# Windowed attention feeding a routed MoE: x turned between the two pairs of turned probabilities, and another tail of the routing

## The reference

```python
scores = scale * np.matmul(q, k.transpose(0, 1, 3, 2))
keep = is_sink | in_window                    # pos < 4, or 0 <= rel < 128
a = softmax(np.where(keep, scores, -1e9))
x = np.matmul(a, v)                           # then [3072 tokens, 512]

logits = x @ w_gate                           # [3072, 8]
expert_idx = np.argmax(logits, axis=1)
gate_w = softmax(logits)[expert_idx]
out[mask] = gate_w[mask, None] * (np.maximum(x[mask] @ w1[e], 0.0) @ w2[e])   # for each expert e

h = out @ w_in
result = (h - np.tanh(h)) @ w_out
```

## Time and profile before

| | us |
|---|---|
| median of three runs | 1124.79 (1124.62 to 1126.35) |
| the profiled execution, whole | 1124.74 |
| its span, first to last instruction | 1123.0 |
| passes of attention, start of the span to the last pass's scores | about 180 |
| tail of the routing, to the first product of stage two | 180 to 203.6 |
| stages two and three | 203.6 to 1123 |
| TensorE busy in the whole span | 1089.1 |

### The profile page before, as it was taken

One profiled execution on the slowest core, in us unless ns is written; L12 is line 12 of the kernel. 1 busy time (PEld: TensorE's weight loads), 2 busy tenths in 40 slices (PEclk: granted clock), 3 DMA queues, 4 the chain that ended last, 5 costly groups with the idle time before them and its releaser, 6 DMA issues.

```text
span 1123.0 us, 17069 instructions
## 1 busy us (share of the span) xinstructions
PE 1089.1 (97%) x5993; PEld 875.9 (78%) x5993; DVE 610.1 (54%) x1326; ACT 478.3 (43%) x1016; POOL 492.7 (44%) x494
## 2 busy tenths in 40 slices
PE   9999998899999999999989999999999999999995
PEld 6777775688888888888867888888888888888884
DVE  6787686222232223223258666666666666666664
ACT  7788874414133414442444333333333333333331
POOL 3256525707025436482274345335335335435432
PEclk9999998999999999999999999999999999999998
DMA  8636723524215344464231100001010010001000
GB/s 274 194 125 211 247 82 123 179 94 161 74 52 192 93 151 141 150 203 144 90 109 58 37 10 38 19 20 39 10 29 38 1 38 38 1 1 38 1 1 38
DMA packets 37916, 99.44 MB, mean 89 GB/s; under 512 B 8272, under 2 KB 8400, under 8 KB 32720
## 3 DMA queue, kind: packets, MB, share of 16 engines
q1 hardware_dynamic: 29392, 52.30, 14.9%
q0 software_dynamic: 8448, 46.17, 11.8%
HBM read 75.84 MB, written 22.61 MB: 88 GB/s over the span
## 4 chain that ended last, share of the span: by engine, by line
PE 91%; DVE 3%; POOL 2%; issue 2%; DMA 1%; ACT 1%; SPq 0%; POOLq 0%; DVEq 0%; ACTq 0%
PE bank L668 22%; PE bank L660 22%; PE bank L596 14%; PE bank L610 14%; PE bank L426 5%; PE bank L460 4%; PE bank L442 3%; PE bank L602 2%; PE bank L583 1%; PE bank L492 1%; DVE x_tok L951 1%; PE bank L648 1%; PE bank L504 1%; POOL sq L1376 1%; DMA qT<-qt 0%
## 5 line engine op out<-in xcount | busy, mean ns | idle before, releaser
L1286 POOL TENSOR_TENSOR weights<-raw,weights 128x1024 fp32r<-128x1024 f32 x72 | 171.3, 2401 | 201.2 <-ACT weights L716 200.0
L660 PE MATMUL bank<-mT_hi,weights 128*128 128x512 f32 x768 | 253.0, 391 | 1.9 <-DVE mT_lo L1113 1.9
L668 PE MATMUL bank<-weights,gT_hi 128*128 128x512 f32 x768 | 241.8, 396 | 6.9 <-DVE gT_lo L1170 6.7
L1375 POOL TENSOR_SCALAR ser<-ser 128x512 f32<-128x512 f32 x96 | 64.0, 666 | 288.1 <-DVE ser L1152 288.0
L668 PEld LDWEIGHTS bank<-weights,gT_hi 128*128 128x128 f32 x768 | 142.2, 189 | 41.1 <-DVE gT_lo L1170 12.7
L660 PEld LDWEIGHTS bank<-mT_hi,weights 128*128 128x128 f32 x768 | 145.0, 189 | 32.4 <-DVE mT_lo L1113 2.1
L668 PE MATMUL bank<-weights,gT_lo 128*128 128x512 f32 x384 | 150.5, 392 | 0.0
L660 PE MATMUL bank<-mT_lo,weights 128*128 128x512 f32 x384 | 150.1, 391 | 0.0
L596 PE MATMUL bank<-weights,mT_hi 128*128 128x512 f32 x464 | 147.8, 400 | 1.5 <-issue 1.5
L610 PE MATMUL bank<-weights,hT_hi 128*128 128x512 f32 x464 | 148.7, 401 | 0.0
L859 ACT ACTIVATE bank<-bank 128x512 f32<-128x512 f32 x96 | 55.9, 582 | 214.0 <-DVE ser L1162 214.0
(11 more groups left out here) (141 smaller groups left out, 1575.6 us busy)
## 6 DMA issues: line engine op xcount, KB each, us to landing
raw<-w_all POOLq DMA_DIRECT2D x32, 1024.0 KB, 5.6
raw<-w_all SPq DMA_DIRECT2D x8, 1024.0 KB, 6.5
sorted_y<-ys SPq DMA_DIRECT2D x30, 257.0 KB, 3.3
xs<-sorted_x SPq DMA_DIRECT2D x29, 257.0 KB, 2.8
kT<-kt SPq DMA_DIRECT2D x24, 264.0 KB, 2.9
qT<-qt SPq DMA_DIRECT2D x24, 256.0 KB, 3.3
v_in<-vt SPq DMA_DIRECT2D x24, 256.0 KB, 3.7
raw<-sorted_y SPq DMA_DIRECT2D x20, 257.0 KB, 2.7
```

Of the source, the lines that this page charges most:

```text
L660: done = e.matmul(bank[HB[n % 3]][:, :], wt[:, f // 2, c, cols], x[:, c, :], start=(c == 0 and m == 0), stop=(c == CH - 1 and m == 2))
L668: done = e.matmul(bank[YB[i]][:, :], x[:, n % 3, rows], wt[:, f, :], start=(f == 0 and m == 0), stop=(f == GCH - 1 and m == 2))
L1286: e.tensor_tensor(lo, src, hi.bitcast(F32), ALU.subtract).then_inc(s_w_lo, 1)
L1375: e.tensor_scalar(row, row, SERIES_2, 1.0, ALU.mult, ALU.add).then_inc(s_ser, 1)
```

## The change

- On TensorE `turn_prob(i, 0)` now stands ahead of `turn_x(w)`, and `turns` follows: `turn_prob(i, 1)` waits for the reader of `turn_prob(i, 0)`, and `turn_x` has its bank from pair 3 of the tile before. VectorE copies `part(i, 0)` ahead of `normalise(w)`.
- The start of each expert's region is added by one more small product in `rank` (`region_b`), not by a step on VectorE; `places` has three steps where it had four.
- The logits are negated when ScalarE copies them, so the maximum becomes a minimum. For the last three sets, of one tile each, `pick` has four steps where it had five, `tally` is left out (`rank` adds the one-hot rows of those tiles by products), and the exponential's sum is taken by ScalarE.
- The ranks of the last three sets have PSUM banks of their own (1, 2, 3), and the logits of the last tile go to bank 6. The wait of `small_bank_read` for them falls away, and `rank` stands where its input is due.
- VectorE's list behind the last pass is written out: the copy of pair 2 first, then `pick`, `gates`, `places` of the single tiles around `add_logits`.
- ScalarE normalises x of the last two tiles, eight activations of 128x64 each with the row's factor as a pointer.
- Of the products that nobody reads, the two are gone, the five stand ahead of the last rank, and 32 stand where 18 stood. Behind the turn of the first slot 11 transposes of the identity are new.

```diff
@@ turns @@
+        if i < ALL:
+            turns += [("prob", i, 0)]
         if 0 <= w < ALL:
             turns += [("x", w, 0)]
         if i < ALL:
-            turns += [("prob", i, 0), ("prob", i, 1)]
+            turns += [("prob", i, 1)]
@@ banks @@
+        def logits_bank(w):
+            return bank[O_BANK] if w == ALL - 1 else bank[R_BANK]
+        def rank_of(b):
+            tiles = SETS[b][1]
+            bk = bank[R_BANK] if b < MULTI else bank[1 + b - MULTI]
+            return bk[:, 0:tiles * E].rearrange("p (t e) -> p t e", t=tiles)
+        def norm_on_act(w):
+            return w >= ALL - 2
@@ tensor: rank @@
+                    for g in range(SETS[MULTI][0], start):
+                        e.matmul(rk, ones[:, :], hot_all[:, g:g + 1, :], start=False, stop=False, skip_group_check=True)
+                e.matmul(rk, ones[:, :], region_b[:, :].unsqueeze(1).broadcast_to([P, tiles, E]),
+                         start=False, stop=True, skip_group_check=True).then_inc(s_rank, 1)
@@ tensor: the passes @@
-                if 0 <= w < ALL:
+                if 0 <= w < ALL - 1:
                     small_bank_read(w)
+                if i == ALL:
+                    rank(MULTI)
                 if 0 <= w < ALL:
                     logits(w)
+                if i < ALL:
+                    turn_prob(i, 0)
+                if 0 <= w < ALL:
                     turn_x(w)
-                if w == ALL - 1:
-                    keep_warm(2)
                 if sinks:
                     sink_values(g)
-                if i < ALL:
-                    turn_prob(i, 0)
+                if i == ALL + 1:
+                    rank(MULTI + 1)
                 if 0 <= w < ALL:
                     turn_logits(w)
-                if i == ALL + 2:
-                    keep_warm(5)
-                if i - 3 in LAST:
-                    rank(LAST.index(i - 3))
+                    if i - 3 in LAST:
+                        rank(LAST.index(i - 3))
+            keep_warm(5, bank[0])
+            rank(MULTI + 2)
...
-            keep_warm(18)
+            keep_warm(32, bank[R_BANK])
@@ tensor: behind the turn of the first slot @@
             turn_slot_x()
+            for _ in range(11):
+                e.transpose(bank[R_BANK][:, 0:P], ident[:, :], ident[:, :])
@@ scalar @@
+            def normalise(w):
+                e.wait_ge(s_rinv, w + 1)
+                e.wait_ge(s_x_turned, w + 1)
+                b = set_of[w - RING_X]
+                e.wait_ge(scattered[b], 16 * SETS[b][1])
+                bk = bank[T_OF[turn_at["x", w, 0] % 2]]
+                for h in range(H):
+                    cols = slice(h * D, (h + 1) * D)
+                    done = e.activation(x_tok[:, w % RING_X, cols], bk[:, cols], ACT.Copy, scale=rinv[:, w % 2, h:h + 1])
+                done.then_inc(s_norm_act, 1)
@@ vector: a pass @@
+                part(i, 0)
-                if 0 <= w < ALL:
+                if w >= 0:
                     normalise(w)
-                if i < ALL:
-                    part(i, 0)
```

More of the change, by code:

```diff
@@ L470, in small_bank_read @@
                 b = next((n for n in range(NSETS) if LAST[n] == w - 2), None)
-                if b is not None:
-                    e.wait_ge(s_place, 3 * b + 1)
+                if b is not None and b < MULTI:
+                    e.wait_ge(s_place, 2 * b + 1)
             def turn_sinks(g):
@@ L1035, in routing_of, with at_once @@
             def routing_of(i):
-                new = LAST.index(i - 3) if i - 3 in LAST else None
-                old = LAST.index(i - 4) if i - 4 in LAST else None
-                if new is not None:
-                    yield from pick(new)
-                if old == NSETS - 1:
-                    e.wait_ge(s_counts, 1)
-                    e.tensor_tensor(tail_rows[:, :], bank[0][:, 0:E], region[:, 0, :], ALU.add).then_inc(s_tail_rows, 1)
-                if old is not None:
-                    yield from places(old)
-                if new is not None:
-                    if new < NSETS - 1:
-                        yield from tally(new)
-                    yield from gates(new)
+                if i - 3 in LAST:
+                    yield from pick(LAST.index(i - 3))
+                if i - 4 in LAST:
+                    yield from places(LAST.index(i - 4))
+                if i - 3 in LAST:
+                    yield from tally(LAST.index(i - 3))
+                    yield from gates(LAST.index(i - 3))
+            def at_once(steps):
+                for _ in steps:
+                    pass
             e.memset(mask[:, :, :, :], 0.0).then_inc(c_zero, 1)
@@ L1054, in vector @@
             e.wait_ge(c_mask0, 1)
-            for i in range(ALL + 4):
+            for i in range(ALL):
                 g, w = i - 1, i - 2
-                in_values = 0 <= g < ALL
                 routing = routing_of(i)
@@ L1062, in vector @@
                     e.wait_ge(c_parted, 2)
-                    e.wait_ge(c_region, 2)
-                if i >= ALL:
-                    for _ in routing:
-                        pass
+                    e.wait_ge(c_region, 3)
                 for h in range(H):
-                    if i < ALL:
-                        masked_max(i, h)
-                    if h == 0 and 0 <= w < ALL:
+                    masked_max(i, h)
+                    if h == 0 and w >= 0:
                         invert(w)
-                    if h == 3 and in_values:
+                    if h == 3 and g >= 0:
                         for p in (2, 3):
@@ L1076, in vector @@
                     next(routing, None)
-                if 0 <= w < ALL:
+                part(i, 0)
+                if w >= 0:
                     normalise(w)
-                if i < ALL:
-                    part(i, 0)
-                if 0 <= w < ALL:
                     add_logits(w)
-                if i < ALL and not part_on_act(i, 1):
+                if not part_on_act(i, 1):
                     part(i, 1)
-                for _ in routing:
-                    pass
-                if i < ALL and i % TILES == 1:
+                at_once(routing)
+                if i % TILES == 1:
                     sink_values_lo(i // TILES)
+            part(ALL - 1, 2)
+            at_once(pick(MULTI))
+            at_once(places(MULTI - 1))
+            at_once(gates(MULTI))
+            at_once(places(MULTI))
+            invert(ALL - 2)
+            add_logits(ALL - 2)
+            at_once(pick(MULTI + 1))
+            at_once(gates(MULTI + 1))
+            invert(ALL - 1)
+            at_once(places(MULTI + 1))
+            add_logits(ALL - 1)
+            at_once(pick(MULTI + 2))
+            at_once(gates(MULTI + 2))
+            at_once(places(MULTI + 2))
+            e.wait_ge(s_counts, 1)
+            e.tensor_tensor(tail_rows[:, :], bank[0][:, 0:E], region[:, :], ALU.add).then_inc(s_tail_rows, 1)
             counts = bank[0][:, 0:E]
```

121 lines of the change are left out of this document (75 added, 46 removed).

## The result

The changed kernel takes 1114.65 us (median of four runs, 1114.19 to 1115.05), the kernel before 1125.07 on the same chip: a ratio of 0.9906 with a 95% interval of 0.9888 to 0.9923. The forecast was 1115.9.

The account below looks back on a forecast made before the run. The chain that ended last was TensorE nearly all the way, so savings count where it waits or is slowed. Passes 3.8 + tail 3.5 + unread products 1.55 = 8.85 off 1124.74 gives 1115.9 us; range 1113.2 to 1119.9.

Parts of the forecast that it names:

- The passes: Attention passes: pair 1 starts 1.25 to 1.27 after pair 0, not 1.51; 16 x 0.24 = 3.8 us, bounds 0 to 4.2.
- Rival A: In the passes another wait replaces the wait for x; all of the 3.8 gone, 1119.7 us; chance 0.13.
- Passes 8 and 14: No gain there: a VectorE routing step beside GpSimd's weight remainder takes 1.05, not 0.2, and holds the next scores' masking.
- The tail: From pass 23 to the last scatter: scatter issued at 190.63 against 194.18; 3.5 us gained after 0.05 for late clearing.
- ScalarE's activations: Tail, x of the last two tiles: one activation 0.28, the next 0.18 behind it, eight 1.55 us.
- GpSimd issues 0.28 after its last input: Tail: the last scatter issues 0.28 after ScalarE's second eight activations end at 190.35, so at 190.63.
- The landing and the load behind the scatter: After the last scatter: the first clearing DMA, for which the load waits, comes up to 0.6 late; 0.05 taken.
- Rival C: Tail: ScalarE's small activations don't overlap, eight take 2.25, the tail gains 2.2; 1117.2 us; chance 0.08.
- Rival E: Slower: ScalarE bounds the tail, 0.688 per activation adds 8.1 and 1.55 is not won; 1125.55 us; chance 0.02.
- The unread products: Start of stage two: 11 transposes hold the clock, 18 products take 4.15, not 5.72; 1.55 us, bounds 0 and 1.6.
- Rival D: Start of stage two: the transposes don't hold the clock, 1.55 not won; 1117.45 us; chance 0.10.
- Rival B: First slot: the 32 products stand in the way, ending 1.65 after the slot is due; 1117.5 us; chance 0.10.

Follow-up runs that it names:

- second execution: The changed kernel itself run and traced once more, nothing changed (after_again): 1114.15 us, ratio 0.9910 to the kernel before.
- split_last: Against the changed kernel, x of the last tile is shared: ScalarE normalises six heads, VectorE the last two; 1116.78 us, ratio 0.9914 to the kernel before.
- x_wait_first: Against the changed kernel, GpSimd's scatters of the last two tiles wait first for ScalarE's x, then dest, gate, ids; 1116.71 us, ratio 0.9913 to the kernel before.

## Why the prediction was right, point by point

**The passes: right in place and count, too small.** The forecast was 16 passes of 0.24 and five of nothing, 3.8 us. The kernel without transposes, whose clock is up in all passes, shows 157.83 - 152.77 = 5.06. Counted from its logits to the next, each of the five passes named (7, 8, 13, 14, 19) gives 0.01 to 0.10, and each of the other 16 gives 0.22 to 0.35, 0.30 in the mean. The term that was mis-sized is the one pass: pair 1 starts 1.22 to 1.26 behind pair 0 in 15 of the 16 (1.35 in pass 12), as worked out, but the stretch before had grown to 1.54 from pass 14 on, and the scores follow pair 1 sooner by 0.03 (0.59 before, 0.56 now, in pass 3). Rival A is excluded as a price: in 14 of the 16 passes pair 1 waits neither for the copy of pair 0 nor for x. In passes 2 and 20 it does wait for the copy, the sign that the prediction named for A, but it starts 1.22 behind pair 0 all the same, and the gain stays.

**Passes 8 and 14** gain 0.04 and 0.05, as the forecast had it. What it did not see is a third collision of VectorE and GpSimd, in pass 13, which makes the way to the logits of pass 14 1.27 longer (9.29 to 8.02).

**The tail: right in its steps, too large.** Forecast 3.55 to the last scatter, measured 17.17 - 14.51 = 2.66. From the turn of the sinks to the last tile's logits it was to be 4.37 us (181.6 to 185.97) and was 4.36; from there to `dest` 4.03, and was 3.99; to the end of ScalarE's activations 4.38, and was 4.47. Two steps failed. The turn of the sinks came 4.87 behind the logits of pass 23 and not 4.59: 0.28. And "GpSimd issues 0.28 after its last input" was taken from a scatter whose last input was `dest`; behind x from ScalarE it is 0.81, by the order of GpSimd's waits: 0.53. With 0.09 for ScalarE these make up the 0.89 missing. (One sum on the way is 0.09 short by its own terms: 181.6 + 0.2 + 2 x 1.02 is 183.84, not 183.75.) The landing and the load behind the scatter, for which the forecast took 0.05 off, cost 0.71 more than before in the profiled execution and 0.11 in the second.

**ScalarE's activations.** Eight take 1.73 us, 0.20 from start to start; I had 1.55, 0.18 apart. Rival C (2.25) is excluded. (The Trainium skill, "ScalarE: Activation LUTs", What ACT_TABLE_LOAD costs, states the terms from which the prediction estimated 2.0: the measurement lies between the two. The sum by that estimate had the tail at 2.7, which came true, but 0.53 of the loss is GpSimd's.) Rival E is excluded. Moving x to ScalarE costs 0.22 as the change has it, and gains 0.30 with ScalarE's x first in GpSimd's list: the place was right, the order of the waits was not.

**The unread products: right.** Forecast 1.55; 18 products went from 5.72 to 4.33 to 4.37 in most executions, which is 1.4, and taking the transposes away costs 1.5. Rival D came true in part, with 4.96, in one execution of eleven that have them or products in their place, the one first profiled. Rival B shows with 44 products, not with 32.

**What balanced it.** The forecast was 1.25 above the median, and that it came so near is in part luck. In the profiled execution the places that it counts, from the first logits to the 19th product of stage two, give 4.11 + 2.66 - 0.71 + 0.33 = 6.39 us of its 8.85. The other 3.25 come from stretches that it leaves out: 0.86 ahead of the first logits, 0.16 in stage two, 2.23 in stage three. In the second execution it is 8.02 and 2.13. The passes give 1.3 more than forecast where the clock holds, the tail 0.9 less. The clock's fall in pass 14, when it comes, takes 0.95 back (153.72 against 152.77 from the first logits to those of pass 23). The start to the first logits varies from 18.32 to 19.52 among the variants. Stage three was 1.6 to 2.4 us shorter than in the one execution of before that was profiled, by where the clock falls.

## What to carry to other kernels

Where two producers fill the same pair of buffers by turns, put the one whose reader is slow where the next wait on its buffer is furthest away; here a swap of two neighbours in the order was worth half of a large change. An estimate of "last input to issue" holds only for the input it was measured on: look at which wait of the list it was, and put the one that comes last in time first in the list. A clock fall seen in one trace is a draw, not a property: before you build on it or blame an edit for it, take a second trace of the same kernel, and look for what the engine would have waited for there: in stage three a fall in the second layer's first group cost nothing, one at the stage's start 1.6 us.

## What the runs showed of the hardware that was not expected

- GpSimd's scatter starts about 0.3 us behind the wait that its code names first, and 0.8 behind any other (0.29 and 0.77 to 0.81; 0.90 in `split_last`, whose list has one wait more).
- VectorE's step of 0.68 us becomes 1.95 beside a GpSimd step of 2.37 that started before it.
- On two of the chips, all seven kernels run there show halts that the others don't: 1.2 us between the first logits and those of pass 13 (78.6, elsewhere 77.4), and about 2.7 in the tail of the six that hold the new tail (7.0 to 7.1 from the turn of the sinks to the last tile's logits, 4.36 elsewhere). VectorE and ScalarE of `x_wait_first` in order of time, where TensorE's products for them had ended by 180.8:

```profile
182.25 0.17 DVE L1075 TENSOR_TENSOR place<-bank,hot_all 128x8 f32<-128x8 f32 x1 [2.90 <-remote]
...
183.73 0.28 ACT L782 ACTIVATE lT<-bank 128x128 f32<-128x128 f32 x1 [4.77 <-remote]
```

  Both engines take up their work 1.8 and 2.9 us late, and the profile names no releaser but "remote", which its chain of waits calls "another core or an unknown queue". Their cause stays open; the kernel before is 1.2 to 2.9 us slower on those chips as well (1126.27 and 1126.65, elsewhere 1123.75 to 1125.07), so the ratios suffer less than the times.
